# Moving items of a hand-written schedule: last-chunk sums, the loads of the second network and one large store

## The chip, the cores and the metric

The kernel runs on one core of a Trainium2 chip. The metric is the device time of one execution in microseconds (us). Each engine of the core (TensorE or PE for matmuls, VectorE or DVE, ScalarE or ACT, GpSimd or POOL, and SyncE or SP, which here only issues DMAs) runs its own instructions strictly in order and meets the others through semaphores.

## The reference

Three stages follow each other. Attention over 4 batches of 8 heads, 576 positions, head size 64, made of a pooled part and a local part; then two token-wise networks on 2304 tokens of 512 features:

```python
def _moe_ref(x, w1, w2, w3, w_out):
    h = np.maximum(np.maximum(x @ w1, x @ w2), x @ w3)      # 512 -> 768
    return (h @ w_out).astype(np.float32)                   # 768 -> 512

def _moe2_ref(x, w_in, w_out):
    h = x @ w_in                                            # 512 -> 2048
    g = np.maximum(0.01 * h, h)
    return (g @ w_out).astype(np.float32)                   # 2048 -> 512
```

The attention result is `out_up + out_local`: softmax attention over means of 4 neighbours, repeated 4 times, plus softmax attention in which a position sees only those less than 4 away.

## The kernel before

All products are made from float32 values split in two: ScalarE rounds a tensor to a high part (`..._hi`), VectorE or GpSimd subtracts to get the low part (`..._lo`), and TensorE adds three products, low times high, high times low, high times high.

The order of the first phase is one list, `FIRST`. `first_phase()` (L135) gives each item a place, a number near the index g of an MLP matmul group `("M", g)`, and sorts by it. Every engine walks the same list and runs its own part of each item, so an item's place is its place in each engine's queue. There are NG1 = 88 groups for the first two thirds of the tokens, in four chunks (22 groups each: 18 "h" groups, three per 128 features of h, then 4 "y" groups); then, for the last 768 tokens, the stage of `("Q", n)`, n = 0 to 9, and the y groups M.88 to M.95. Matmul groups and attention jobs share PSUM banks: a job waits until the one before it in its bank has been evacuated (`begin`, L916).

The items that matter here:

- Attention of a unit u: D (group sums), S (scores), E (exponentials), G (sums of v on GpSimd, L840), N (normalise on VectorE, L1595), T (transposes, L975), V (values on TensorE, combine on VectorE, L1619). LR loads v's rows. `plan` gives for each u the places of N and G, T, S of u + 2, and V. `("W", c, step)` splits weights: ScalarE L1397, GpSimd L851.
- M.g (h groups): maxima of three products; `h_high` and `h_low` (L1311, L1656) of the chunk's last h tile run in the item of the first y group, M.84 for the last such chunk. The y groups are evacuated to one of two `y_out` buffers by ScalarE (`mlp`, L1378; `last_y`, L1369 for M.88 on), which waits for the DMA store of two groups before, and SP stores them to `y_dram` (`store_y`, L755).
- The h of the last 768 tokens is made by a fast matrix product of 7 products instead of 8 per pair of blocks. XS.0 (VectorE, L1680) makes the sums of x, XS.1 to XS.7 their high and low parts (ScalarE L1317, VectorE L1689). LS (SP, L735) loads raw weights; LS.0 and LS.1 wait for the seventh low part. WS.0 makes the weight sums of the first quad: four GpSimd operations into the one buffer `ws_sums` (L873), then `ws_hi` on ScalarE (L1324) and `ws_lo` on VectorE (L1694). `("Q", n)` multiplies quad n in the order 0, 3, 6, 2, 1, 5, 4 (`last_quad`, `last_product`), and makes the weight sums of quad n + 1; ScalarE's part of Q.n begins with `ws_hi` of n + 1 and then copies the first banks.
- The second network: LX loads token blocks, B and X2 make their sums and parts, LU.q loads the raw weights of quad q (`load_quad`, L707), U.q makes sums and parts of them into `u_even` or `u_odd` (`quad_sums` L859 on GpSimd, `quad_high` L1415, `quad_low` L1765), LO and O load and split the output weights. `store_quad(q)` (L716) stores the finished u buffer, 1792 KB, to DRAM for use with the next tokens. After `FIRST` comes a loop over quads (L795 for SP): products 0 to 6, with slices of M.95 between them in the first quad. Product 1 of the first quad waits for M.93's evacuation, product 2 for ScalarE's first copy (L1461).

Of the kernel before, what the change touches and what calls it, by code (L numbers as in the profile page):

```python
# [16 lines left out]
B, H, S, D = 4, 8, 576, 64  # L17
# [90 lines left out]
NG1 = NC1 * NM  # L108
# [26 lines left out]
def first_phase():  # L135

    items = []

    def put(at, *names):
        for name in names:
            items.append((at, len(items), name))

    put(0, ("LQ", 0), ("LQ", 1), ("LR", 0), ("LQ", 2), ("LV", 0), ("LR", 1), ("LQ", 3), ("LV", 1), ("WL", 0),
# [7 lines left out]
    for i in range(NF1):  # L155
        put(4, ("WL", NF1 + i))
    for c, at in ((2, 0.5), (3, 2.4), (4, 5.4), (5, 8.4)):
        put(at, ("W", c, 0))
        put(at + 1, ("W", c, 1))
    for c, at in ((6, 10.3), (7, 11.3), (8, 12.7), (9, 13.7), (10, 14.7), (11, 15.7)):  # L160
        put(at, ("W", c, 0))
    put(0, ("LQ", 4))
    put(1.2, ("S", 5), ("E", 5))
    put(1.5, ("LQ", 5))


    plan = {4: (2, 5.2, 6.2, 7.7), 5: (6.4, 9, 10, 11.6), 6: (10.2, 12.8, 13.8, 15.6), 7: (13.9, 16.4, 18.3, 19.6),
# [3 lines left out]
    for u, (n_at, t_at, s_at, v_at) in plan.items():  # L171
        p, part = UNITS[u]
        if part == WHOLE:
            put(n_at - 2, ("LR", p))
            put(n_at, ("G", p))
        put(n_at, ("N", u))
        put(t_at, ("T", u))
        if s_at is not None:
            put(s_at - 1.5, ("D", u + 2))
            put(s_at, ("S", u + 2))  # L180
            put(s_at + 0.5, ("E", u + 2))
            q = UNITS[u + 2][0]
            if u + 2 >= WHOLE0 and q + 2 < NPAIR:
                put(s_at + 0.4, ("LQ", q + 2))
        put(v_at, ("V", u))
        if u + 2 < NU:
            put(v_at, ("LV", u + 2))
    for c in range(1, NC1):

        for kk in range(KM):  # L190
            put(NM * (c - 1) + HG + (2.3 if c == 1 and kk == KM - 1 else 1), ("X", c, kk))

    put(NG1 - 11, ("XS", 0))
    for n in range(NP):
        put(NG1 - 10.5 + 0.5 * n, ("XS", n + 1))
    put(NG1 - 7, ("LS", 0), ("LS", 1))
    put(NG1 - 4.5, ("WS", 0))

    for n in range(SQ + 1):
        put(NG1 + n, ("Q", n))  # L200
        if n + 2 < SQ:
            put(NG1 + n + 0.5, ("LS", n + 2))


    y0 = NG1 + SQ + 1
    put(y0 - 1.5, ("LX", 0))
    put(y0 - 0.1, ("LU", 0))
    put(y0 + 0.2, ("B", 0), ("X2", 0, 0), ("X2", 0, 1))
    put(y0 + 1.2, ("X2", 0, 2), ("LO", 0), ("LO", 1))
    put(y0 + 2.2, ("X2", 0, 3), ("U", 0))  # L210
    put(y0 + 3.2, ("X2", 0, 4), ("X2", 0, 5), ("LU", 1))
    put(y0 + 4.2, ("X2", 0, 6), ("LO", 2), ("LO", 3))
    put(y0 + 6.2, ("U", 1), ("O", 0), ("O", 1))

    for g in range(NG):
        put((g if g < NG1 else y0 + g - NG1) + 0.001, ("M", g))
    return [name for _, _, name in sorted(items, key=lambda item: item[:2])]


FIRST = first_phase()  # L220


# [116 lines left out]
def build(nc, kq, v_sum, v_band, w123, w_out, v_in, v_out, out, y_dram, u_dram):  # L339
    with ExitStack() as ctx:  # L340
# [292 lines left out]
        def u_of(quad):  # L633
            return (u_even, u_odd)[quad % 2]
# [28 lines left out]
        def _(sp):  # L663
# [3 lines left out]
            def load_kq(p):  # L667
                if p >= PAIRS:

                    sp.wait_ge(att_done, JOB["sl1", p if p < PAIRS + 2 else p + 2] + 1)  # L670
                sp.dma_start(kq_of(p), kq[divmod(p, PAIRS)]).then_inc(kq_loaded[p % PAIRS], 16)

            def load_v_rows(p):
                if p >= 2:
                    sp.wait_ge(vmean_ready, p - 1)
                sp.dma_start(v_rows[:, p % 2], v_sum[divmod(p, PAIRS)]).then_inc(v_loaded[p % 2], 16)

            def load_v_windows(u):
                p, part = UNITS[u]
                lo, hi = PART_V[part]  # L680
                if u >= 2:
                    sp.wait_ge(att_done, JOB["av1", u - 2] + 1)
                sp.dma_start(v_win[:, u % 2, lo:hi, :], v_band[divmod(p, PAIRS)][:, lo:hi, :]
                             ).then_inc(vwin_loaded[u % 2], 16)

            def weights(c):
                src = w123[c] if c < NF1 else w_out[(c - NF1) * P:(c - NF1 + 1) * P, :]
                sp.dma_start(w_place(w_raw, c), src).then_inc(w_loaded[c], 16)
# [27 lines left out]
            def store_quad(q):  # L716
                sp.wait_ge(u_split, q + 1)
                sp.dma_start(u_dram[q], u_of(q)[:, :].bitcast(F32)).then_inc(u_stored[q % 2], 16)
# [9 lines left out]
            def load_second(f):  # L728
                if f == 0:
                    sp.wait_ge(s_done, S_ALL)  # L730
                if f == FIRST_O:
                    sp.wait_ge(mlp_done, NG)
                sp.dma_start(o_place(f)[2], v_out[f * P:(f + 1) * P, :]).then_inc(o_loaded[f], 16)

            def load_quad_raw(n):  # L735
                fp, w = divmod(n, 3)
                if n < 2:

                    sp.wait_ge(xs_split, NP)
                else:  # L740
                    sp.wait_ge(ws_ready, 4 * (n - 1))
                for i in range(2):
                    src = w123[2 * fp + i].rearrange("p (k w e) -> p w k e", w=3, e=P)
                    sp.dma_start(ws_raw[:, n % 2, i], src[:, w]).then_inc(ws_loaded[n % 2], 16)
# [22 lines left out]
            for item in FIRST:  # L767
                if item[0] == "LQ":
                    load_kq(item[1])
                elif item[0] == "LR":  # L770
                    load_v_rows(item[1])
                elif item[0] == "LV":
                    load_v_windows(item[1])
                elif item[0] == "WL":
                    weights(item[1])
                elif item[0] == "M" and item[1] != NG - 1:
                    store_y(item[1])
                elif item[0] == "LS":
                    load_quad_raw(item[1])
                elif item[0] == "LX":  # L780
                    load_tokens(item[1])
                elif item[0] == "LU":
                    load_quad(item[1])
                elif item[0] == "LO":
                    load_second(item[1])
# [9 lines left out]
            for quad in range(NQT):  # L795
                c, q = divmod(quad, NQ)
                if c == 0:
                    if q + 2 < NQ:
                        load_quad(q + 2)
                        load_second(2 * (q + 2))  # L800
                        load_second(2 * (q + 2) + 1)
                    if q == 0:
                        store_y(NG - 1)
                        store_quad(0)
                    if q + 1 < NQ:
                        store_quad(q + 1)
                if quad + 1 >= NQ and quad + 1 < NQT:
                    reload_quad(quad + 1)
                if c and q == 0:
                    store_outputs(c - 1)  # L810
                if q == 1 and c + 1 < NCH:
                    load_tokens(c + 1)
# [1116 lines left out]
```

## Time and profile before

| | us |
|---|---|
| median of 3 runs | 785.99 (785.85 to 786.02) |
| profiled execution | 786.02 |
| its span, first to last instruction | 784.2 |
| PE busy | 766.0 (98%) |
| DVE busy | 446.6 (57%) |
| ACT busy | 293.4 (37%) |
| POOL busy | 158.5 (20%) |

The span is what the profile's positions count from. Matmuls overlap, so that the start-to-start distance, not the duration, is the pace. "Idle before, and whose work ended it" is given in square brackets in the timelines; a DMA row of SP (SPq) is the issue, not the transfer.

### The profile page before, as it was taken

The numbers are of one execution on the slowest core, as the hardware profiler recorded it, in microseconds if no ns is written. First come the engines' busy times: TensorE is split into PE (matmuls) and PEld (weight loads), VectorE is DVE, ScalarE is ACT, GpSimd is POOL, SyncE is SP. The second block draws the span as 40 slices with busy tenths as digits, with TensorE's granted clock in tenths as the row PEclk, the third lists the DMA queues.
The fourth block names the chain that finished last, engine by engine and source line by source line (L and its number), as shares of the span: only waits on it lengthen the run. The fifth ranks groups of instructions, "written<-read, shape, count | busy, mean of one in ns | idle before, by whom it ended". The sixth has DMA issues, their size and how long they took to land.

```text
span 784.2 us, 13517 instructions
## 1 busy us (share of the span) xinstructions
PE 766.0 (98%) x5416; PEld 686.6 (88%) x5416; DVE 446.6 (57%) x777; ACT 293.4 (37%) x689; POOL 158.5 (20%) x204
## 2 busy tenths in 40 slices
PE   8899999999999989999999999999999999999998
PEld 7688899988888878999988888889989898989886
DVE  6679588577645561666946556564434466334333
ACT  4474534432343232433544434452222244222222
POOL 4588121111102012441243354110000000000000
PEclk9999999999999999999999999999999999999999
DMA  8452333322121013212358455446243226322402
GB/s 294 142 205 73 127 102 117 112 67 80 54 85 38 1 53 103 83 54 81 118 194 335 171 214 216 172 145 219 102 157 117 94 94 228 134 94 95 149 39 81
DMA packets 37630, 98.91 MB, mean 126 GB/s; under 512 B 2880, under 2 KB 23360, under 8 KB 34496
## 3 DMA queue, kind: packets, MB, share of 16 engines
q1 hardware_dynamic: 37568, 98.05, 35.8%
q8 instruction: 43, 0.70, 0.4%
q14 instruction: 19, 0.16, 0.1%
HBM read 73.92 MB, written 24.12 MB: 125 GB/s over the span
## 4 chain that ended last, share of the span: by engine, by line
PE 86%; DVE 4%; issue 1%; ACT 1%; DMA 1%; POOL 1%; SPq 0%; DVEq 0%; ACTq 0%
PE mlp_ps L1047 9%; PE mlp_ps L1049 8%; PE mlp_ps L1048 8%; PE mlp_ps L1199 7%; PE mlp_ps L1201 7%; PE mlp_ps L1200 7%; PE att_ps L1220 6%; PE att_ps L1222 6%; PE att_ps L1221 6%; PE mlp_ps L1222 3%; PE mlp_ps L1221 3%; PE mlp_ps L1220 3%; PE att_ps L1119 2%; PE att_ps L1121 2%; PE att_ps L1120 2%; PE att_ps L1036 1%
## 5 line engine op out<-in xcount | busy, mean ns | idle before, releaser
L1047 PE MATMUL mlp_ps<-x_hi,wa_lo 128*128 128x288 f32 (+1 forms) x288 | 101.6, 353 | 1.2 <-DVE h_raw L1678 1.2
L1049 PE MATMUL mlp_ps<-x_hi,wa_hi 128*128 128x288 f32 (+1 forms) x288 | 97.5, 338 | 0.0
L1048 PE MATMUL mlp_ps<-x_lo,wa_hi 128*128 128x288 f32 (+1 forms) x288 | 97.1, 337 | 0.0
L1488 ACT ACTIVATE h_hi<-wa_raw 128x384 fp32r<-128x384 f32 x72 | 37.6, 524 | 102.9 <-DVE wa_raw L1822 101.7
L1820 DVE TENSOR_TENSOR wa_raw<-mlp_ps,h_raw 128x384 f32<-128x384 f32 x24 | 13.4, 558 | 85.1 <-PE mlp_ps L1201 54.6
L1047 PEld LDWEIGHTS mlp_ps<-x_hi,wa_lo 128*128 128x128 f32 x288 | 54.1, 188 | 7.3 <-DVE h_raw L1678 1.4
L1049 PEld LDWEIGHTS mlp_ps<-x_hi,wa_hi 128*128 128x128 f32 x288 | 54.1, 188 | 4.6
L1048 PEld LDWEIGHTS mlp_ps<-x_lo,wa_hi 128*128 128x128 f32 x288 | 54.2, 188 | 4.0
L1834 DVE TENSOR_TENSOR h_lo<-wa_raw,h_hi 128x384 fp32r<-128x384 f32 x72 | 45.0, 631 | 22.4 <-ACT h_hi L1488 20.4
L1220 PE MATMUL att_ps<-wa_hi,h_lo 128*128 128x512 f32 x132 | 52.4, 397 | 1.0 <-DVE h_lo L1834 1.0
L846 POOL TENSOR_TENSOR v_rows<-v_rows 72x512 f32<-72x512 f32 x16 | 22.1, 1382 | 153.7 <-DMA v_rows<-in_v_sum 153.7
L1222 PE MATMUL att_ps<-wa_hi,h_hi 128*128 128x512 f32 x132 | 52.2, 396 | 0.0
L1221 PE MATMUL att_ps<-wa_lo,h_hi 128*128 128x512 f32 x132 | 52.1, 395 | 0.0
L1047 PE MATMUL mlp_ps<-h_hi,wo_lo 128*128 128x288 f32 (+1 forms) x96 | 34.0, 354 | 4.6 <-DVE h_lo L1660 4.6
L1467 ACT ACTIVATE half_max<-mlp_ps 128x384 f32<-128x384 f32 x48 | 23.5, 491 | 29.3 <-PE mlp_ps L1201 29.3
L1199 PE MATMUL mlp_ps<-early_hi,u_even 128*128 128x384 f32 x96 | 32.9, 342 | 0.7 <-ACT half_max L1467 0.7
L1049 PE MATMUL mlp_ps<-h_hi,wo_hi 128*128 128x288 f32 (+1 forms) x96 | 32.9, 343 | 0.0
L1048 PE MATMUL mlp_ps<-h_lo,wo_hi 128*128 128x288 f32 (+1 forms) x96 | 32.8, 342 | 0.0
L1199 PE MATMUL mlp_ps<-early_hi,u_odd 128*128 128x384 f32 x96 | 32.8, 342 | 0.0
L1201 PE MATMUL mlp_ps<-early_hi,u_odd 128*128 128x384 f32 x96 | 32.7, 340 | 0.0
L1201 PE MATMUL mlp_ps<-early_hi,u_even 128*128 128x384 f32 x96 | 32.7, 340 | 0.0
L856 POOL TENSOR_TENSOR wa_lo<-wa_raw,wa_hi 128x192 fp32r<-128x192 f32 x48 | 29.5, 647 | 15.0 <-ACT wa_hi L1400 15.0
(211 smaller groups left out, 2021.6 us busy)
## 6 DMA issues: line engine op xcount, KB each, us to landing
u_even<-u_scratch SPq DMA_DIRECT2D x8, 1792.0 KB, 7.4
u_odd<-u_scratch SPq DMA_DIRECT2D x8, 1792.0 KB, 7.4
kq_in<-in_kq SPq DMA_DIRECT2D x14, 576.0 KB, 3.8
u_scratch<-u_even SPq DMA_DIRECT2D x4, 1792.0 KB, 8.6
u_scratch<-u_odd SPq DMA_DIRECT2D x4, 1792.0 KB, 9.3
v_rows<-in_v_sum SPq DMA_DIRECT2D x16, 288.0 KB
wa_raw<-in_w SPq DMA_DIRECT2D x6, 768.0 KB, 5.6
v_win<-in_v_band SPq DMA_DIRECT2D x12, 384.0 KB, 3.6
```

What stands on the lines that cost most here:

```text
L856: nc.gpsimd.tensor_tensor(lo[:, n, :], raw[:, n, :], hi[:, n, :].bitcast(F32), ALU.subtract).then_inc(w_lo_done, 1)
L1047: nc.tensor.matmul(ps, wlo, xhi, start=(n == 0), stop=False)
L1048: nc.tensor.matmul(ps, whi, xlo, start=False, stop=False)
L1049: last = nc.tensor.matmul(ps, whi, xhi, start=False, stop=(n == len(pairs) - 1))
L1199: nc.tensor.matmul(ps, wlo[:, k], xhi[:, k], start=(first and k == 0), stop=False, skip_group_check=True)
L1200: nc.tensor.matmul(ps, whi[:, k], xlo[:, k], start=False, stop=False, skip_group_check=True)
L1201: last = nc.tensor.matmul(ps, whi[:, k], xhi[:, k], start=False, stop=(k == KT - 1), skip_group_check=True)
L1220: nc.tensor.matmul(ps, glo, hi, start=(f == 0), stop=False)
L1221: nc.tensor.matmul(ps, ghi, lo, start=False, stop=False)
L1222: last = nc.tensor.matmul(ps, ghi, hi, start=False, stop=(f == NF2 - 1))
L1488: nc.scalar.activation(g_tile(h_hi, quad, part), g_raw[part], ACT.Copy).then_inc(g_hi_ready, 1)
L1834: nc.vector.tensor_tensor(g_tile(h_lo, quad, part), g_raw[part], g_tile(h_hi, quad, part).bitcast(F32), ALU.subtract).then_inc(g_split, 1)
```

## The change

Places in the list, and one store moved from the loop into it:

- Unit 8's N (and G.4 with it, and LR.4 two places earlier) goes from 15.8 to 15.2. The order was V.6 (15.6), W.11 (15.7), G.4, N.8; it is G.4, N.8, V.6, W.11.
- XS.0 to XS.7 go from 77 to 80.5 (before M.77 to before M.81) to 77.5 to 84.5, one after each group (XS.7 after M.84). LS.0 and LS.1 go from 81 (before M.81) to 85.5 (after M.85), WS.0 from 83.5 (after M.83) to 86.5 (after M.86).
- y0 is 98. LU.0 goes from just before M.88 to just after it, with LO.0 and LO.1 right behind it (they were after M.89). U.0 stays after M.90, with LU.1 (was after M.91) and the new item SU.0, `store_quad(0)`, right behind it; X2.3 goes from before U.0 to after M.91, with X2.4; X2.5 and X2.6 are after M.92; U.1 goes from after M.94 to after M.93.
- `store_quad(0)` leaves the loop, where it followed M.95's store.

```diff
-            8: (15.8, 20.4, 21.4, 23.4), 9: (21.7, 24.7, 25.7, 27.7), 10: (26.2, 29.5, 30.5, 32.5), 11: (31.2, 34.5, 35.5, 37.5),
+            8: (15.2, 20.4, 21.4, 23.4), 9: (21.7, 24.7, 25.7, 27.7), 10: (26.2, 29.5, 30.5, 32.5), 11: (31.2, 34.5, 35.5, 37.5),
...
-    put(NG1 - 11, ("XS", 0))
+    put(NG1 - 10.5, ("XS", 0))
     for n in range(NP):
-        put(NG1 - 10.5 + 0.5 * n, ("XS", n + 1))
-    put(NG1 - 7, ("LS", 0), ("LS", 1))
-    put(NG1 - 4.5, ("WS", 0))
+        put(NG1 - 9.5 + n, ("XS", n + 1))
+    put(NG1 - 2.5, ("LS", 0), ("LS", 1))
+    put(NG1 - 1.5, ("WS", 0))
...
     put(y0 - 1.5, ("LX", 0))
-    put(y0 - 0.1, ("LU", 0))
-    put(y0 + 0.2, ("B", 0), ("X2", 0, 0), ("X2", 0, 1))
-    put(y0 + 1.2, ("X2", 0, 2), ("LO", 0), ("LO", 1))
-    put(y0 + 2.2, ("X2", 0, 3), ("U", 0))
-    put(y0 + 3.2, ("X2", 0, 4), ("X2", 0, 5), ("LU", 1))
-    put(y0 + 4.2, ("X2", 0, 6), ("LO", 2), ("LO", 3))
-    put(y0 + 6.2, ("U", 1), ("O", 0), ("O", 1))
+    put(y0 + 0.2, ("LU", 0), ("LO", 0), ("LO", 1), ("B", 0), ("X2", 0, 0), ("X2", 0, 1))
+    put(y0 + 1.2, ("X2", 0, 2))
+    put(y0 + 2.2, ("U", 0), ("LU", 1), ("SU", 0))
+    put(y0 + 3.2, ("X2", 0, 3), ("X2", 0, 4), ("LO", 2), ("LO", 3))
+    put(y0 + 4.2, ("X2", 0, 5), ("X2", 0, 6))
+    put(y0 + 5.2, ("U", 1))
+    put(y0 + 6.2, ("O", 0), ("O", 1))
...
+                elif item[0] == "SU":
+                    store_quad(item[1])
...
                     if q == 0:
                         store_y(NG - 1)
-                        store_quad(0)
```

## Rows read from the trace of the kernel before

**Rows 1.** The page, part 1: busy us (share of the span) xinstructions
```profile
PE 766.0 (98%) x5416; PEld 686.6 (88%) x5416; DVE 446.6 (57%) x777; ACT 293.4 (37%) x689; POOL 158.5 (20%) x204
```
**Rows 2.** Waits of PE: waiting tile <- releaser: us in total, times, longest
```profile
PE mlp_ps L1047 <- DVE h_lo L1660: 4.6, 2, 2.6
```
**Rows 3.** Timeline of PE, 73 to 80: start us, us, what, [idle before]
```profile
73.76 0.44 PE L997 MATMUL att_ps<-ident,prob_l 128*128 128x128 f32 x2
...
79.84 0.40 PE L1047 MATMUL mlp_ps<-h_hi,wo_lo 128*128 128x288 f32 x1 [2.04 <-DVE h_lo L1660]
```
**Rows 4.** Timeline of DVE, 73 to 77 us
```profile
73.12 0.46 DVE L1648 TENSOR_TENSOR x_raw<-att_ps,upT 128x116 f32<-128x116 f32 x2 [0.92 <-ACT upT L1299]
...
75.65 0.81 DVE L1616 TENSOR_TENSOR prob_l<-prob_l,row_inv 128x640 f32<-128x640 f32 x1
```
**Rows 5.** Timeline of POOL, 73 to 76 us and at 248 us
```profile
73.68 1.43 POOL L856 TENSOR_TENSOR wo_lo<-wo_raw,wo_hi 128x256 fp32r<-128x256 f32 x2 [0.56 <-ACT wo_hi L1400]
75.07 2.90 POOL L846 TENSOR_TENSOR v_rows<-v_rows 72x512 f32<-72x512 f32 x1
...
248.76 1.28 POOL L846 TENSOR_TENSOR v_rows<-v_rows 72x512 f32<-72x512 f32 x1 [10.23 <-DMA v_rows<-in_v_sum]
```
**Rows 6.** Windows: us, PE, PEld, DVE, ACT, POOL busy, PEclk, DMA share, GB/s
```profile
80.00:85.00 5.00, 5.00 (x63) 4.53 (x64) 3.22 (x4) 2.26 (x11) 0.00 (x0) 0.66 0.44 142
295.00:300.00 5.00, 5.00 (x25) 4.28 (x23) 0.00 (x0) 1.04 (x2) 2.31 (x4) 1.00 0.15 52
```
**Rows 7.** Timeline of SP, 283 to 309 us: DMA issues
```profile
283.98 2.67 SPq L744 DMA_DIRECT2D ws_raw<-in_w  x4
296.20 12.14 SPq L764 DMA_DIRECT2D y_scratch<-y_out  x4
```
**Rows 8.** Timeline of POOL at 288 us: first of four such operations
```profile
288.73 0.74 POOL L880 TENSOR_TENSOR ws_sums<-ws_raw 128x256 f32<-128x256 f32 x1 [37.88 <-DMA ws_raw<-in_w]
```
**Rows 9.** Timeline of ACT, 291 to 309 us
```profile
291.71 1.06 ACT L1329 ACTIVATE ws_hi<-ws_sums 128x1024 fp32r<-128x1024 f32 x1 [7.52 <-POOL ws_sums L885]
...
308.83 0.48 ACT L1341 ACTIVATE s_tmp<-att_ps 128x384 f32<-128x384 f32 x1
```
**Rows 10.** Timeline of DVE at 292 us
```profile
292.80 1.23 DVE L1696 TENSOR_TENSOR ws_lo<-ws_sums,ws_hi 128x1024 fp32r<-128x1024 f32 x1 [3.23 <-ACT ws_hi L1329]
```
**Rows 11.** Timeline of PE: end of M.84's wait, start of Q.0, its third product
```profile
294.65 0.48 PE L1047 MATMUL mlp_ps<-h_hi,wo_lo 128*128 128x480 f32 x1 [2.56 <-DVE h_lo L1660]
...
307.22 0.34 PE L1119 MATMUL att_ps<-xs_hi,wa_lo 128*128 128x384 f32 x1
...
309.37 0.44 PE L1119 MATMUL att_ps<-xs_hi,ws_lo 128*128 128x384 f32 x1
```
**Rows 12.** Timeline of SP, 376 to 381 us
```profile
376.28 0.38 SPq L713 DMA_DIRECT2D u_raw<-in_w_in  x1
380.03 0.36 SPq L753 DMA_DIRECT2D y_scratch<-y_out  x1
```
**Rows 13.** DMA issues, 376 to 378 us: KB each, median us to landing
```profile
u_raw<-in_w_in SPq DMA_DIRECT2D x1, 512.0 KB, 3.5
```
**Rows 14.** DMA issues, 407 to 410 us: the first large store
```profile
u_scratch<-u_even SPq DMA_DIRECT2D x1, 1792.0 KB, 5.9
```
**Rows 15.** DMA issues, 420 to 425 us: four loads right behind a large store
```profile
blocks<-y_scratch SPq DMA_DIRECT2D x4, 384.0 KB, 9.3
```
**Rows 16.** Timeline of ACT, 396 to 400 us
```profile
396.42 0.49 ACT L1376 ACTIVATE y_out<-mlp_ps 128x384 f32<-128x384 f32 x1 [2.69 <-PE mlp_ps L1049]
396.81 1.05 ACT L1424 ACTIVATE u_odd<-u_sums 128x1024 fp32r<-128x1024 f32 x1
...
399.62 0.47 ACT L1467 ACTIVATE half_max<-mlp_ps 128x384 f32<-128x384 f32 x1
```
**Rows 17.** Timeline of PE: product 2 of quad 0, first outputs of quad 1
```profile
400.24 0.41 PE L1199 MATMUL mlp_ps<-early_hi,u_even 128*128 128x384 f32 x1 [0.70 <-ACT half_max L1467]
...
425.88 0.50 PE L1220 MATMUL att_ps<-wa_hi,h_lo 128*128 128x512 f32 x1 [0.34 <-DVE h_lo L1834]
```

## The prediction

> **What bounds the kernel now.** I read the page's busy times first. TensorE is busy 98% of the span, the next engine 57% [rows 1], so all that an edit of the order can give or take is idle time of TensorE, some 18 us in all, plus what its clock does. Second comes the view of TensorE's waits: the largest is for `h_lo` (L1660), two waits, 4.6 us together [rows 2]. Third, the timelines of the stretches that the diff touches say what each engine did at these waits. The diff touches three: A, unit 8's preparation (near 75 us); B, the sums of the last chunk (270 to 310 us); C, the passage to the second network (376 to 400 us). No arithmetic changes; every engine runs its items in order, so what counts is who is queued behind whom.
>
> **A: N.8 and G.4 ahead of V.6 and W.11.** TensorE waits 2.04 us before 79.84 [rows 3]. VectorE is late there: after the combine of unit 6 (73.12) it normalises unit 8 until 76.4 [rows 4], and only then comes the work that feeds `h_lo`. It idled 0.9 us before that combine, so with N.8 first its chain ends 0.9 us sooner. But the combine now waits for N.8, some 3 us of VectorE work, and ends near 75.3. T.7's transposes, at 73.76 [rows 3], use the bank that the combine empties: TensorE stands there 1.6 us. On GpSimd G.4 now precedes W.11, whose last part the first y group waits for: G.4 takes 1.28 to 2.90 + 0.72 us, W.11 1.43 [rows 5], from about 73.1, so the y group starts at 76.6 to 78.2 by GpSimd and at 77.3 by the transposes, against 75.6 now, and reaches the matmul that now starts at 79.84 between 79.3 and 80.2, with nothing left to wait for. A is worth -0.5 to +0.4; I take 0: the wait is moved, not removed.
> The Trainium skill ("SBUF — State Buffer", Who interferes with whom) says that a VectorE operation with two SBUF inputs and a GpSimd one that reads SBUF exclude each other, the first to start holding the port. The trace agrees (2.90 us beside VectorE, 1.28 alone [rows 5]). By the rule G.4, which would now start first, would push N.8 back 0.9 us, and A would be +0.6 instead of 0.
>
> **The clock.** After the 2.04 us pause the granted clock fell to 0.66 in 80 to 85 us, at most 1.7 us lost; after the 2.56 us pause near 294 it stayed at 1.00 [rows 6]. With A's pause cut in two I expect this fall to go, -1.7.
>
> **B: XS, LS, WS later.** Now WS.0 stands before M.84 in ScalarE's and VectorE's order, and M.84 carries the last `h_hi`/`h_lo` of the chunk; GpSimd's sums come only when the loads land, so TensorE waits 2.56 us before 294.65 [rows 11]. With WS.0 after M.86 this goes: -2.7 with the slow first matmul. The spreading of XS over eight groups costs nothing: VectorE has its sums and subtractions beside MLP groups of 2.6 us each, and the last that matters, XS.6 (0.95 us) ahead of h_low, lies under the 3.3 us of y matmuls that don't need it.
> What is late next: the LS loads. They were issued at 283.98; now they stand in SP's queue behind M.85's store, and XS.7 too is behind M.84's evacuation (it ends near 295, before that). The y stores begin at 296.20 [rows 7], a group apart; a group is 18 matmuls of 0.22 us, 4.0 us (57 matmuls from 294.65 to 307.22 [rows 11]). M.85's is at 296.2 + 4.0 - 2.7 = 297.5, the first LS load at 297.8. GpSimd started 4.75 us after the issue (283.98 to 288.73) [rows 7, 8]: 302.6. Four sums of 0.74 us, ScalarE's 1.06 and VectorE's 1.23 take it from there to 294.03, 5.3 us [rows 8 to 10]: `ws_lo` is ready at 307.9. The Q stage begins at 307.22 - 2.7 = 304.5; its first product takes 6 x 0.175 = 1.05 us, its second needs this `ws_lo`: a pause of 2.35 us. Then it gets worse, since ws_sums has one buffer: GpSimd can't make the second quad's sums before 307.9. They end at 311.0 (0.14 + 4 x 0.74), ScalarE must make ws_hi of them (0.95 to the next start) before it may copy the first bank, and 0.54 us after that copy starts TensorE goes on (308.83 to 309.37) [rows 9, 11]: 312.5, where it was 309.37. That is +3.1 net of the 2.7 gained, and a second pause of 3.5 us. Ends: +1.5, if the loads reach GpSimd in the 3.5 us of another 512 KB load [rows 13] instead of 4.75 (1.25 less, and a little for a quieter VectorE), and +4.
> I expect the clock to fall after this longer pause, +1.7 at the price of [rows 6]; with A's fall gone the clock is 0 net.
> The Trainium skill ("TensorE: Matmul & The Clock Gate", HAM oscillation) says that a long pause of the matmuls is followed by matmuls at 1.2 instead of 2.4 GHz, each time. The trace bears that out after 2.04 us and not after 2.56. By the page the fall at Q is sure, and one at C likely too, which gives the dearer rival below.
>
> **C: the order after y0.** LU.0 was issued at 376.28, before M.88's store (380.03) [rows 12]; now it stands behind it, at 380.4. It lands after 3.5 us [rows 13], the sums end near 387.1 (VectorE's crowding of GpSimd is gone), U.0's three roundings and subtractions near 390.5; still ahead of 396.2 where TensorE needs them. LU.1 follows at 390.5 and right behind it, new here, SU.0: 1792 KB, which land 5.9 us after issue with free queues [rows 14]. M.91's store is queued behind that. What that means the trace shows once: 384 KB loads behind such a store took 9.3 us [rows 15]. SU.0 goes out at 390.9, 512 KB are ahead of it (some 1.5 us): it lands near 398.3, M.91's store near 398.8. M.93's evacuation on ScalarE waits for M.91's store (same y_out buffer), and product 1 of the first quad waits for M.93's evacuation: it could start at 397.8 and starts at 399.5. Behind that evacuation ScalarE has U.1's roundings, M.94's evacuation and O.0, O.1: the same work that now lies between 396.42 and the copy at 399.62, 3.2 us [rows 16]. The copy begins at 402.5, product 2 0.6 us later at 403.1, against 400.24 [rows 16, 17]: +2.9. A gain comes back: the store of u_even is over when ScalarE wants the buffer, so the next load and sums are early and don't crowd VectorE before 425.88, whose 0.34 us and slow first matmul go [rows 17]: -0.5. C is +2.4. Ends: -1.3 (both waits gone) and +4.
> From there to the end TensorE has no idle time that the change touches, so nothing hides or gives back the sum.
>
> **Sum.** The profiled execution took 786.02 us (span 784.2, 1.8 around it), the median of the runs is 785.99: one number. 786.0 + 0 (A) + 3.1 (B) + 2.4 (C) + 0 (clock) = 791.5.
>
> **Rivals.**
> 1. Only one of B and C costs what I say. If the engines of the DMA serve small stores beside the large one, C is about 0: 789.1. For it: loads and stores use different ends of the memory. Against: [rows 15]. Or B is at its low end: 789.9. With the clock fall gone and none new, 787.4. Chance 0.18.
> 2. Dearer clock: the falls at Q and at C both come, or A's stays: +1.7 each, 793.2 to 794.9. For it: B's two pauses, 2.35 and 3.5 us, have 1.05 us of matmuls between them. Chance 0.2.
> 3. Faster: the loads for Q are in time. It turns at SP: were the LS loads issued by 294.7 (3.1 us before my 297.8), the Q stage would be level with now; by 291.9 it would have no pause, and B gives its 2.7. If also SU.0 does no harm and the waits at 400.24 and 425.88 go (-0.8, -0.5) and A's fall of the clock, the time is 786.0 - 5.7 = 780.3. For it: SP has nothing to do between 284 and 296, and the gap at 294.65 is surely removed. Against: SP takes its items in order, and M.85's output can't exist before 296.5. Chance 0.12.
> 4. It nets out: low ends of B and C, 785 to 787. Chance 0.05.
>
> **How the numbers follow.** My forecast has 0.45; its own range is 790 to 793. The range 787.0 to 795.0 takes in rivals 1 and 2 and leaves out 3, 4 and a rest above 795. What a measurement can tell from no change is 0.2%, 1.6 us: faster is rival 3, 0.12; same is rival 4, 0.05; slower is the rest, 0.83.
>
> **What would show it.** In the trace after: the wait for `h_lo` (L1660) near 292 gone (B's gain); the ws_raw loads issued after the second y store, GpSimd's first ws_sums near 302; TensorE waiting for `ws_lo` (L1696) some 2.3 us and for `s_tmp` (L1341) some 3.5 us at the start of Q; a fall of the clock just behind it and none near 82; T.7's transposes waiting for the combine (L1648) 1.6 us; a ScalarE wait for the y_scratch store near 393 to 399, and product 1 and product 2 late. I am wrong if the ws_raw loads go out before 295, or if the small stores land within 3 us of their issue although SU.0 is ahead.

## The result and the profile after

The changed kernel takes 794.21 us (median; 792.54 to 798.31 in 4 runs) where the kernel before took 786.00 on the same chip (785.85 to 787.81, 4 runs): a ratio of 1.0107, 95% interval 1.0065 to 1.0148. It is slower, by some 8 us. The profiled execution took 792.95 us, its span 791.2, 7.0 longer than before. Lines below L780 are one or two further down than in the kernel before.

The page, part 1, busy time and share: TensorE has 2.9 us more than before [rows 1] for the same 5416 matmuls, so they ran slower; the rest of the 7 us is idle time.

```profile
PE 768.9 (97%) x5416; PEld 690.5 (87%) x5416; DVE 443.0 (56%) x777; ACT 294.0 (37%) x689; POOL 153.8 (19%) x204
```

TensorE's waits (waiting tile, releaser, total, times, longest). The two `h_lo` waits of [rows 2] are gone and four others head the list:

```profile
PE mlp_ps L1200 <- ACT y_out L1377: 3.4, 1, 3.4
PE att_ps L1120 <- ACT s_tmp L1342: 3.2, 1, 3.2
PE att_ps L998 <- DVE x_raw L1649: 2.7, 2, 2.2
PE att_ps L1120 <- DVE ws_lo L1697: 1.6, 1, 1.6
```

**A.** The timelines of GpSimd, VectorE and TensorE (start us, us, what, [idle before]):

```profile
71.86 1.27 POOL L847 TENSOR_TENSOR v_rows<-v_rows 72x512 f32<-72x512 f32 x1
...
72.24 1.50 DVE L1615 TENSOR_TENSOR prob_g<-prob_g,row_inv 72x576 f32<-72x576 f32 x1
...
74.40 0.45 DVE L1649 TENSOR_TENSOR x_raw<-att_ps,upT 128x116 f32<-128x116 f32 x2
...
74.81 0.41 PE L998 MATMUL att_ps<-ident,prob_l 128*128 128x128 f32 x2 [2.21 <-DVE x_raw L1649]
```

N.8 is now ahead of the combine, and T.7's transposes wait 2.21 us for the combine instead of M's matmul waiting 2.04 us [rows 3]. Two products ahead of this place and behind it show what A is worth. V.6 and V.7 before, then after:

```profile
70.88 0.45 PE L1013 MATMUL att_ps<-probT_g,v_mean 72*64 72x57 f32 x8
...
85.90 0.45 PE L1013 MATMUL att_ps<-probT_g,v_mean 72*64 72x57 f32 x8
```

```profile
69.65 0.45 PE L1014 MATMUL att_ps<-probT_g,v_mean 72*64 72x57 f32 x8
...
84.62 0.45 PE L1014 MATMUL att_ps<-probT_g,v_mean 72*64 72x57 f32 x8
```

The first 1.23 us arose ahead of V.6. The run of A alone, with the same edit, has V.6 at 71.28, so they are chance of one execution and no effect of it; between the two marks the change is -0.05 us. G.4 took 1.27 us where it took 2.90 [rows 5], and N.8's first operation with two inputs in SBUF 1.50 where it took 0.90 before:

```profile
74.82 0.90 DVE L1614 TENSOR_TENSOR prob_g<-prob_g,row_inv 72x576 f32<-72x576 f32 x1
```

That is the port rule that the prediction quotes from the Trainium skill ("SBUF — State Buffer", Who interferes with whom): the first to start holds the port; the trace agrees. VectorE's 0.6 us of lateness do show in the wait, 2.21 us where 1.6 were forecast, but the whole stretch is level, so they did not make A +0.6.

**B.** The timelines again: SP's issues, GpSimd's first sum (4.2 us after the loads' issue), VectorE's `ws_lo`, TensorE's first stop (a wait of TensorE), ScalarE's second `ws_hi`, TensorE's second stop:

```profile
292.09 4.27 SPq L764 DMA_DIRECT2D y_scratch<-y_out  x2
296.40 2.67 SPq L744 DMA_DIRECT2D ws_raw<-in_w  x4
...
300.59 0.73 POOL L881 TENSOR_TENSOR ws_sums<-ws_raw 128x256 f32<-128x256 f32 x1 [51.24 <-DMA ws_raw<-in_w]
...
304.66 1.23 DVE L1697 TENSOR_TENSOR ws_lo<-ws_sums,ws_hi 128x1024 fp32r<-128x1024 f32 x1 [10.87 <-ACT ws_hi L1330]
...
305.94 0.45 PE L1120 MATMUL att_ps<-xs_hi,ws_lo 128*128 128x384 f32 x1 [1.60 <-DVE ws_lo L1697]
...
308.98 1.06 ACT L1330 ACTIVATE ws_hi<-ws_sums 128x1024 fp32r<-128x1024 f32 x1 [3.90 <-POOL ws_sums L886]
...
310.47 0.69 PE L1120 MATMUL att_ps<-xs_hi,ws_lo 128*128 128x384 f32 x1 [3.19 <-ACT s_tmp L1342]
```

The order is the predicted one to the step: loads behind two y stores, first sum, split, stop; second sum only when the one buffer is free, second stop. The wait of M.84 [rows 11] is gone, so that Q.0 starts at 303.11.

**C.** The timelines: SP's issues near 394 us, ScalarE behind them, and TensorE at products 1 and 2 of quad 0:

```profile
394.21 0.37 SPq L713 DMA_DIRECT2D u_raw<-in_w_in  x1
394.62 0.50 SPq L718 DMA_DIRECT2D u_scratch<-u_even  x1
395.17 0.43 SPq L753 DMA_DIRECT2D y_scratch<-y_out  x1
...
403.54 0.49 ACT L1377 ACTIVATE y_out<-mlp_ps 128x384 f32<-128x384 f32 x1 [7.03 <-DMA y_scratch<-y_out]
...
404.17 0.66 PE L1200 MATMUL mlp_ps<-early_hi,u_even 128*128 128x384 f32 x1 [3.42 <-ACT y_out L1377]
407.74 0.41 PE L1200 MATMUL mlp_ps<-early_hi,u_even 128*128 128x384 f32 x1 [0.41 <-ACT half_max L1468]
```

The DMA issues of 395.1 to 395.6 us (KB each, us from issue to landing):

```profile
u_scratch<-u_even SPq DMA_DIRECT2D x1, 1792.0 KB, 8.3
y_scratch<-y_out SPq DMA_DIRECT2D x1, 192.0 KB, 8.3
```

A store of 192 KB takes 8.3 us with 1792 KB ahead of it; issued just ahead of them, in a run further down, it took 4.4. The Trainium skill ("DMA: Bandwidth & Descriptors", Queues, rings and completion order) says that each DMA engine takes the descriptors of one queue in ring order; the row agrees.

**The clock.** Windows (us, busy time and count of PE, PEld, DVE, ACT and POOL, granted clock, DMA share, GB/s). The fall behind A's wait is still there, a window earlier than in [rows 6], and there are two new ones, behind the stops of B and C:

```profile
75.00:80.00 5.00, 5.00 (x28) 5.00 (x27) 2.98 (x5) 0.83 (x2) 1.73 (x3) 0.66 0.00 0
80.00:85.00 5.00, 5.00 (x81) 4.35 (x80) 3.17 (x4) 2.40 (x11) 0.00 (x0) 1.00 0.41 142
...
310.00:315.00 5.00, 4.53 (x14) 4.53 (x15) 1.46 (x2) 1.29 (x4) 2.83 (x4) 0.50 0.36 107
...
405.00:410.00 5.00, 4.59 (x21) 4.17 (x20) 3.36 (x5) 3.08 (x7) 3.23 (x4) 0.79 0.54 176
```

The same matmuls, before and after, give the 7 us of span: ahead of A -1.23, A -0.05, B +4.08 (product 6 of quad 9 at 375.02 before, first row, and 377.82 after, second row), C +4.19 (the matmul of [rows 17] at 425.88 is at 432.87, third row, and 2.80 of these 6.99 us were there already).

```profile
375.02 0.34 PE L1119 MATMUL att_ps<-xs_hi,wa_lo 128*128 128x384 f32 x1
```

```profile
377.82 0.34 PE L1120 MATMUL att_ps<-xs_hi,wa_lo 128*128 128x384 f32 x1
...
432.87 0.48 PE L1221 MATMUL att_ps<-wa_hi,h_lo 128*128 128x512 f32 x1
```

### The profile page after: what moved, and what is told of

The parts are those of the page before. It is cut to its first block, busy times and chain, and to the rows that moved or that the text cites. A ratio compares the mean times of both kernels' runs of the same rounds, so it can differ in the third digit from the quotient of the medians.

```text
span 791.2 us, 13517 instructions
## 1 busy us (share of the span) xinstructions
PE 768.9 (97%) x5416; PEld 690.5 (87%) x5416; DVE 443.0 (56%) x777; ACT 294.0 (37%) x689; POOL 153.8 (19%) x204
## 4 chain that ended last, share of the span: by engine, by line
PE 87%; DMA 2%; DVE 2%; POOL 1%; ACT 1%; issue 1%; SPq 0%; ACTq 0%; DVEq 0%; POOLq 0%
PE mlp_ps L1048 9%; PE mlp_ps L1050 8%; PE mlp_ps L1049 8%; PE mlp_ps L1200 7%; PE mlp_ps L1202 7%; PE mlp_ps L1201 7%; PE att_ps L1221 6%; PE att_ps L1223 6%; PE att_ps L1222 6%; PE mlp_ps L1223 3%; PE mlp_ps L1222 3%; PE mlp_ps L1221 3%; PE att_ps L1120 2%; PE att_ps L1122 2%; PE att_ps L1121 2%; PE att_ps L1037 1%
## 5 line engine op out<-in xcount | busy, mean ns | idle before, releaser
L1221 PE MATMUL att_ps<-wa_hi,h_lo 128*128 128x512 f32 x132 | 52.4, 397 | 0.6 <-DVE h_lo L1835 0.6
L1201 PE MATMUL mlp_ps<-early_lo,u_even 128*128 128x384 f32 x96 | 32.8, 341 | 0.0
```

The lines of the kernel that those rows point to most:

```text
L1201: nc.tensor.matmul(ps, whi[:, k], xlo[:, k], start=False, stop=False, skip_group_check=True)
L1221: nc.tensor.matmul(ps, glo, hi, start=(f == 0), stop=False)
```

## The experiments

Times are medians; a ratio is to the kernel before on the same chip, with its 95% interval; "worth" is that ratio less 1, times 786 us.

### The three parts alone

The edit of each is the part of the diff that its name says: unit 8's `15.8` to `15.2`; the XS, LS and WS places; the list from y0 on with the large store in the list.

> The kernel before with part A alone (unit 8's N and G.4 earlier). Theory: the wait is moved from the y group to T.7's transposes and the clock's fall moves with it, so the time is that of before, 786.0 within 0.5. Rival: A's cut wait costs 1 us or more of the 8 (787 or above), or loses its clock fall (784.3).

> The kernel before with part B alone (XS, LS, WS later). Theory: the 2.7 us of the old wait are gained, two pauses of 1.6 and 3.2 us with their restarts come at the start of the Q stage, and a fall of the clock adds 2: +4.1 us, 790.1. Rival 1 (waits only, the clock is chance of one execution): +2.4, 788.4. Rival 2 (B is not the cause, C is nearly all): 786 to 787.

> The kernel before with part C alone (loads and large store of the second network). Theory: product 1 of the first quad waits for M.93's evacuation, which waits for M.91's small store queued behind the large one; with a fall of the clock +4.2 us, 790.2. Rival: without B's shift the small store lands in time, +1 or less.

A alone: 786.65 us, 1.0006 (0.9994 to 1.0017), worth nothing; the 2.2 us wait for `x_raw` is there. The fall behind it is not in this profile: V.6 to V.7 is 13.74 us (71.28 to 85.02), where the same stretch with the wait for `h_lo` and no fall is 13.5 in five other runs: level to 0.2 us without the fall, as it is to 0.05 with it. B alone: 789.44, 1.0038 (1.0023 to 1.0053), +3.0, between the +4.1 expected and the +2.4 of its rival. C alone: 790.97, 1.0066 (1.0044 to 1.0089), +5.2. The three sum to 1.0110, the whole is 1.0107 (1.0065 to 1.0148): within these intervals no effect of one part on another shows.

### C without the store's move, and the store's move alone

```diff
-    put(y0 + 2.2, ("U", 0), ("LU", 1), ("SU", 0))     # C, here without SU:
+    put(y0 + 2.2, ("U", 0), ("LU", 1))
```

> Part C alone, but the large store stays in the loop where it was. Theory (the large store is C's cost): product 1 isn't late, product 2 about 1 us late because LU.0 and so U.1 are: 786.0 to 787.2. Rival (LU.0 behind M.88's store is C's cost, the large store harmless): about 790, as the run with the store moved.

```diff
-    put(y0 + 2.2, ("X2", 0, 3), ("U", 0))             # before, here with SU:
+    put(y0 + 2.2, ("X2", 0, 3), ("U", 0), ("SU", 0))
```

> The kernel before with only the large store of quad 0's scratch moved to y0+2.2 (into the stage's list, behind U.0), every load where it was. If part C is a sum of two costs, the late u loads (2.6 us by the run of C without the store's move) and the store standing ahead of the y stores (the rest of C's 4.4), this gives +1.8 to +2. Rival one, that the store costs only because the late LU.1 puts it right behind other loads: 0. Rival two, that the store now also stands ahead of LU.1 and delays the second sums: +3 or more.

Without the store's move: 789.25, 1.0036 (1.0021 to 1.0051), +2.8, outside the 786.0 to 787.2 expected. I had given the late load too little. The store's move alone, every load where it was: 793.68, 1.0088 (1.0072 to 1.0103), +6.9, more than C alone by the medians, though the intervals overlap. Timelines of this last kernel, SP, GpSimd and TensorE:

```profile
390.73 0.33 SPq L718 DMA_DIRECT2D u_scratch<-u_even  x1
391.10 0.43 SPq L753 DMA_DIRECT2D y_scratch<-y_out  x1
391.57 0.95 SPq L713 DMA_DIRECT2D u_raw<-in_w_in  x1
...
399.95 0.74 POOL L867 TENSOR_TENSOR u_sums<-u_raw 128x256 f32<-128x256 f32 x1 [13.01 <-DMA u_raw<-in_w_in]
...
406.39 0.66 PE L1200 MATMUL mlp_ps<-early_hi,u_even 128*128 128x384 f32 x1 [5.47 <-ACT half_max L1468]
```

With LU.1 left at y0+3.2 the store is ahead of this load too, and the load reaches GpSimd 8.4 us after its issue. That is rival two of the expectation. C moves LU.1 ahead of the store and so avoids the dearest form of its own edit.

### C with LU.0 early, and C with the store later

```diff
-    put(y0 + 0.2, ("LU", 0), ("LO", 0), ("LO", 1), ...
+    put(y0 - 0.1, ("LU", 0))
+    put(y0 + 0.2, ("LO", 0), ("LO", 1), ...
```

> Part C (the changed order of the second stage's loads and quad 0's scratch store) with one thing put back: the load LU.0 at y0-0.1, a step earlier than in part C. Theory, that the lateness of LU.0 pushes the split of U.0, and with it LU.1 and the large store, back: these come 1.3 to 3 us sooner and the time falls from part C's +5.2 to +2.5 to +4. Rival, that the y store behind the large store is the whole cost wherever that stands: +5 stays.

```diff
-    put(y0 + 2.2, ("U", 0), ("LU", 1), ("SU", 0))
+    put(y0 + 2.2, ("U", 0), ("LU", 1))
+    put(y0 + 3.1, ("SU", 0))
```

> Part C with the large store one step later, at y0+3.1, so that the y store which ScalarE waits 7.0 us for is issued ahead of it. Theory, that this one y store behind the 1792 KB is what the store's move costs: the time is that of part C without the store's move, +2.6 to +2.8. Rival, that the next y stores and the load of the next stage's operands then stand behind it and cost the same a step later: +5 or more.

LU.0 early: 788.82, 1.0018 (1.0005 to 1.0031), +1.4, less than the +2.5 to +4 expected. The store a step later: 791.95, 1.0064 (1.0047 to 1.0081), +5.0; the theory falls. In its trace the y store that ScalarE needed first is ahead of the large one, lands 4.4 us after its issue, in time for product 1, and the next y evacuation stands for a store behind the large one (first row), with TensorE at product 2 behind that (second row):

```profile
401.73 0.49 ACT L1378 ACTIVATE y_out<-mlp_ps 128x384 f32<-128x384 f32 x1 [1.70 <-DMA y_scratch<-y_out]
...
403.78 0.66 PE L1201 MATMUL mlp_ps<-early_hi,u_even 128*128 128x384 f32 x1 [4.22 <-ACT half_max L1469]
```

In both places of the store the y store that comes next is the one that is late. These kernels have clock falls at different places of their spans, so what C does is best read inside one stretch, from the start of quad 0's product 0 to that of its product 2 (starts from each timeline, one execution of each):

| kernel | product 0 | product 1 | product 2 | 0 to 2 | over before |
|---|---|---|---|---|---|
| before | 396.22 | 397.79 | 400.24 | 4.02 | |
| loads late, no store (C without SU) | 397.99 | 399.56 | 403.90 | 5.91 | +1.9 |
| store, LU.0 early | 397.49 | 399.99 | 403.56 | 6.07 | +2.05 |
| C | 396.07 | 400.53 | 404.10 | 8.03 | +4.0 |
| C, store at y0+3.1 | 396.23 | 397.80 | 403.78 | 7.55 | +3.5 |
| store alone, LU.1 behind it | 397.60 | 399.17 | 406.39 | 8.79 | +4.8 |
| the whole change | 399.02 | 404.17 | 407.74 | 8.72 | +4.7 |

The late LU.0 (1.9) and the store ahead of the y stores (2.05) sum to C's 4.0. LU.0's lateness acts through LU.1, which may only be issued when U.0 has been split: its issue is 6.9 us ahead of product 0 in the kernel before (389.35 and 396.22), 7.3 with LU.0 early, 5.5 in C (390.57), and 5.1 with the loads late and no store (392.91 and 397.99).

The table ends where product 2 starts; what a fall of the clock does behind it comes on top. From product 2 to product 4 it is 3.24 us before (400.24 to 403.48) and 3.25 in C alone, and 4.77 in C without the store's move, 5.90 with the store a step later and 5.69 with the store alone, each with a fall there. So by these traces the store's move alone costs 4.8 us by its waits and 2.4 by the clock, close to the +6.9 measured. C alone has no fall in this stretch, and its profiled execution, 789.34, is the fastest of its five; the 4.0 us of the table are the waits only, the +5.2 is from all five.

### B with its load earlier, and B with TensorE kept busy

```diff
-    put(NG1 - 2.5, ("LS", 0), ("LS", 1))
+    put(NG1 - 3.4, ("LS", 0), ("LS", 1))
```

> Part B (the changed order of XS, LS and WS) with the loads' step LS one step earlier still, ahead of M.85, so that its transfers are issued some 2.6 us sooner. If B costs because the small load stands behind the large store of its queue and its sums come late, the two waits (1.6 and 3.2 us) shrink by about that much and the time is 0 to +1 us against before. Rival, that B costs by the place of the splits on ScalarE and not by the load: as B alone, +3.

```diff
+                        fill(9)     # quad 0, ahead of product 3, the first that waits for ws_lo
...
+                        fill(17)    # quad 0, ahead of product 2
```

> Part B with matmuls whose result nobody reads put on TensorE into the two waits at Q's start (9 ahead of the first product that needs ws_lo, 17 ahead of product 2). If the fall of the granted clock behind those waits costs about 2 us and is due to TensorE standing still, the time is 1 to 2 us below part B alone (787.5 to 788.5 against 789.4) and the granted clock of 305 to 315 us is near 1. Rival, that the clock has no share in it: as part B alone or up to 1 us slower, since the fillers can end later than the waits.

LS a step earlier: 786.93, 1.0005 (0.9995 to 1.0016), worth +0.4: B costs nothing then. The issue is at 295.02, 9.3 us ahead of Q.0's start (304.32) where it is 6.7 us ahead in the whole change. The wait for `ws_lo` is gone and the one for `s_tmp` is 2.65 us, since the second sums still need the one buffer. With the fillers (matmuls whose result is not used; the order in quad 0 is product 0, 3, 2): 787.91, 1.0010 (0.9996 to 1.0023), 1.5 us under B alone by the medians and 2.2 by the ratios. Windows of B alone and, in the second fence, of B with fillers:

```profile
310.00:315.00 5.00, 4.12 (x14) 4.12 (x15) 1.23 (x2) 1.70 (x4) 2.83 (x4) 0.54 0.35 107
```

```profile
310.00:315.00 5.00, 4.70 (x27) 4.54 (x27) 2.34 (x3) 1.29 (x4) 2.88 (x4) 1.00 0.38 110
```

Product 2 starts 7.4 us after product 0 in both (303.44 to 310.88, and 303.08 to 310.46), so the fillers hide no wait. From there to the next quad it is 5.94 us in B alone (310.88 to 316.82) and 4.31 with fillers (310.46 to 314.77), 4.27 in the kernel before (309.37 to 313.64). The fall of the clock costs 1.6 us here, by a comparison in which the fillers are the only difference of the two kernels.

### What the waits of the kernel before are worth

```diff
-    put(NG1 - 4.5, ("WS", 0))
+    put(NG1 - 3.5, ("WS", 0))
```

> The kernel before with one step moved earlier: the sums of the scale loads, WS.0, at NG1-3.5 instead of the start of the stage, so that their 2.6 us wait at Q's start (PE for h and w operands) has nothing to wait for. If that wait is on the path and its cause is the lateness of the loads' sums alone, the time is 2.6 to 2.7 us below before (783.3 against 786.0). Rival: what PE saves there is late again at the next operand, and the time is within 0.5 us of before.

```diff
-            8: (15.8, 20.4, 21.4, 23.4), ...
+            8: (18.05, 20.4, 21.4, 23.4), ...
```

> The kernel before with N.8 (and G.4) of the first stage four matmul units later than before, where its operands are there. It takes away the 2.0 us wait of TensorE and, if the clock fall that follows comes from it, that too: 2 to 3.7 us below before (782.3 to 784). Rival, that the wait only moves to the next product that needs x_raw or h_lo, as in unit 8 alone: within 0.5 us of before.

WS.0 a step later in the list, its loads where they were: 782.69, 0.9950 (0.9933 to 0.9967), -3.9. The notion of part B, to get WS.0 out of M.84's way, is right; B spoils it by moving the loads too. N.8 later instead of earlier: 783.62, 0.9961 (0.9948 to 0.9973), -3.1: both the 2.04 us wait and the fall behind it are gone. (The expectation of the first says "earlier" and "Q's start"; the edit puts WS.0 later in the list, and the wait that it takes away is M.84's. N.8 is three groups later, behind M.18, and not four. And B has no large store, of which the expectation of the run with LS a step earlier speaks: there the loads stand behind M.85's store.)

How often the clock falls behind these two waits can be read off the runs together, since most of them leave one or both places as they were. From V.6 to V.7, with the 2.04 to 2.06 us wait for `h_lo` between them, five traces have 15.02 to 15.05 us and a fall (before, C alone, C without the store's move, B with fillers, the store alone) and five have 13.53 to 13.55 and none (B alone, WS.0 late, LS earlier, and C with LU.0 early or the store later). N.8 late has 11.50. So the wait is worth 2.0 us, and the fall, in half of the traces, 1.5. From the end of M.84's wait to Q.0 the kernel before has 12.57 us and C alone 12.58, without a fall; the six others that have this wait (2.05 to 2.45 us) have 14.11 to 14.14, with one. This is the window behind M.84's wait in C without the store's move, where [rows 6] has 1.00:

```profile
295.00:300.00 5.00, 5.00 (x17) 4.19 (x17) 0.00 (x0) 0.57 (x1) 2.40 (x4) 0.66 0.14 52
```

The profile of the kernel before, from which the prediction was made, is thus one of the two without the fall at M.84. With six falls in eight at 1.55 us each, WS.0 late would be worth 1.2 us beyond the 2.7 of the wait with its slow first matmul; this is an estimate from single traces, and it fits the -3.9.

### Both, and the roundings of the second network's first blocks

```diff
-            8: (15.8, 20.4, 21.4, 23.4), ...
+            8: (18.05, 20.4, 21.4, 23.4), ...
...
-    put(NG1 - 4.5, ("WS", 0))
+    put(NG1 - 3.5, ("WS", 0))
...
+    put(y0 + 5.2, ("OH", 0), ("OH", 1))     # ScalarE's part of O, ahead of U.1
     put(y0 + 6.2, ("U", 1), ("O", 0), ("O", 1))
...
-                elif item[0] == "O":            # in ScalarE's walk of the list
+                elif item[0] == "OH":
```

> Three moves on the kernel before together: N.8 and G.4 at 18.05 (2.8 us gained alone), WS.0 at NG1-3.5 (3.7 us gained alone), and ScalarE's part of the second stage's first high halves (O on ScalarE) ahead of U.1, which should take away the 0.85 us that TensorE waits there. If the gains are independent, as the parts of the change were, the sum is 7 us: 779 (778 to 781). Rival, that part of both gains is the clock of the same stretch or that what is saved early is waited for at the next load: 782 to 783, as the better of the two alone.

780.84 us (779.69 to 781.81), 0.9927 (0.9914 to 0.9939): 5.9 us faster than the kernel before and the fastest of all. The ratios of the two single moves give -7.0 together (-5.4 to -8.6 by their intervals), the whole is -5.7 (-4.8 to -6.8), a little short of the 779 expected: they add up within the intervals. TensorE's waits: both `h_lo` waits and the `half_max` wait [rows 17] are gone, and one behind them has grown from 0.6 us (0.8 in each of the two single moves) to 1.4:

```profile
PE att_ps L963 <- ACT prob_g L1256: 2.1, 1, 2.1
PE att_ps L1221 <- DVE h_lo L1835: 1.4, 1, 1.4
PE att_ps L963 <- DVE kq_sum L1555: 1.4, 1, 1.4
```

A new wait of 0.35 us for VectorE has come at product 3 as well. From product 0 to the first output matmul (L1221) it is 13.76 us here (391.48 to 405.24) and 13.52 with WS.0 late alone (392.67 to 406.19), so by these traces the third move gave back all of its 0.7 us and 0.2 more. What it is worth alone was not tried.

## Why the prediction was right, step by step

791.5 was forecast, 794.2 measured, inside the range 787 to 795, though not in the forecast's own 790 to 793, and one of the four runs took 798.3. The profiled execution is 1.45 us above the forecast: -1.23 lies ahead of the edits (one execution's chance), so the steps were 2.7 us too cheap. That it is not more is partly luck: B's waits came 0.7 us cheaper, while the clock (2.1) and C (1.8) came dearer. (The chances in the prediction sum to 1 with nothing left for the rest above 795.)

- **A, 0: right**, by the run of A alone too. The wait moved to T.7's transposes: 2.2 us, not the 1.6 forecast, and no wait for `h_lo` is left behind it.
- **B's waits, +3.1: +2.4 measured.** Q.0 starts 2.8 us sooner relative to the marks (2.7 forecast), the stops are 1.60 and 3.19 us (2.35 and 3.5 forecast). The loads reached GpSimd in 4.2 us and not in 4.75. The cause is shown: with the loads one step sooner the cost is gone. The gain of 2.7 for M.84's wait was read from a trace without a fall behind it; where the fall comes it is 1.5 more. The +4.08 between the marks of one pair of executions, less 1.2 for six falls in eight, is 2.9 by estimate, beside the +3.0 of the runs.
- **The clock, 0 net: this term failed.** A's fall was expected to go with the wait "cut in two"; the wait was not cut but moved, and in the profiled execution the fall moved with it (0 instead of -1.7). Nor was it a fixed cost of the kernel before: it is in half of the traces with the old wait. The fall at Q came, at 2.1 us in this execution (310.47 to 316.82 is 6.35, 4.27 before) and 1.7 in B alone; 1.7 was forecast. One wait of 0.28 us at 317.08 in the kernel before went. Rival 2, the dearer clock, was in this the better case, though the third fall, at C, cost nothing: product 2 waits for ScalarE anyway (product 1 to product 2 is 3.57 us with the fall and without it, in C alone).
- **C, +2.4: +4.2 measured.** The mechanism was right (M.91's store behind the large one, ScalarE, products 1 and 2) and the size off. M.91's store took 8.3 us from its issue at 395.17; I had it landed at 398.8, 2.6 us behind the start of product 0; ScalarE went on at 403.54, 4.5 us behind it, of which 0.9 is LU.1's and the large store's later issue (LU.1 4.8 us ahead of product 0 and not 5.7). The term that I set to nothing, LU.0 behind M.88's store, is worth 1.9 us by itself: ScalarE stood 3.9 us for U.0's sums, which I had as "still ahead of 396.2", true for product 0, but not for LU.1 and the store, which follow U.0's split. The gain at 425.88 is there: 0.5 us (that matmul is 6.99 us later where quad 0's first output matmul, 409.53 before, is 7.49 later).
- **Rival 1** (small stores served beside the large one) is out by the 8.3 us. Its reason, about loads and stores, did not bear on it: the large transfer and the small one are both stores. **Rival 3** gave the right test, "were the LS loads issued by 294.7, the Q stage would be level with now": they were issued at 295.02 in the run with LS earlier, and the time was level.

What stays open: runs of one kernel are spread over 1 to 6 us on one chip, and falls of the clock, some 1.5 us each, can be part of it. After the same wait near 79 us the fall is in the profiled execution before (0.66 in 80 to 85 us), and in B alone, with the same code there, it is not (1.00):

```profile
80.00:85.00 5.00, 4.63 (x71) 4.04 (x72) 3.44 (x5) 2.17 (x10) 0.00 (x0) 1.00 0.39 118
```

What decides between the two no run here shows, and one profile of each kernel gives only the rough shares above (5 of 10, 6 of 8), not how often it happens in one kernel.

## What to carry to other kernels

An item that moves in a hand-written order moves all that it issues: part B moved the splits, which was worth -3.9 us, and with them the loads, which turned it into +3.0. Before a large store is put into a queue, look at which small transfer comes next behind it and who waits for that one; moving the store a step later only chose another victim here. A load that is "in time" for its first reader can still make the next load late, if that one may only be issued when the reader has released its buffer. And one profiled execution can lack a cost that others have: the fall at M.84 is missing from the one that the prediction read and is in six of the seven other traces with that wait.

## What the hardware did that I had not expected

- Waits of TensorE and the granted clock behind them, one execution each: 3.2 us (B alone and the whole change), 3.4 us (the whole change, at C), 4.2 us (C with the store later) and 5.5 us (the store alone) all had a fall to about half, with matmuls 0.32 us apart instead of 0.17; 2.59 us (C without the store's move) and 2.65 us (B with LS earlier) had one and 2.7 us (C alone) none; M.84's wait of 2.05 to 2.56 us had one in six traces of eight, and the 2.04 us at the place of A in five of ten. Where a fall was on the path it cost 1.4 to 2.7 us. The Trainium skill ("TensorE: Matmul & The Clock Gate", HAM oscillation) has the fall behind each long pause; for those of 3.2 us and more the traces here agree, and for the shorter ones they show it in some executions and not in others.
- Matmuls that nobody reads are worth their place: 26 of them in two waits took 1.6 us off B by the trace, in which they shorten no wait.
- A 192 KB store behind 1792 KB landed after 8.3 us, and a 512 KB load behind the same reached its first reader after 8.4 us. Elsewhere such a load landed in 3.5 us [rows 13], and the y stores of the kernel before, between 376 and 405 us (its DMA issues), in:

```profile
y_scratch<-y_out SPq DMA_DIRECT2D x7, 192.0 KB, 2.0
```
